# One engine makes the third unit's outputs, one hidden tile goes to the readout's bank, and the fourth unit's preparation stands further on

## What is computed

```
for t in range(S):
    C = f_stab * C + i_stab * outer(v_t, k_t)
    n = f_stab * n + i_stab * k_t
    y_t = sigmoid(o_gate_t) * (C q_t) / max(|n . q_t|, 1)
...
h = x @ w_in
g = where(h >= 1, h, where(h <= -1, 0, (h + 1)**2 / 4))
x = g @ w_out
...
out += P[:, e:e+1] * (max(x @ w1[e], 0) @ w2[e])
```

## Time and profile before

| | us |
|---|---|
| median of 3 runs (lowest, highest) | 923.47 (922.88, 923.96) |
| the profiled execution | 923.94 |
| span of its instructions | 921.8 |
| TensorE busy | 914.6 |
| VectorE busy | 594.1 |
| ScalarE busy | 464.6 |
| GpSimd busy | 617.8 |

### The profile page before, as it was taken

How to read it: one execution, slowest core, us unless ns; L and a number is a source line. 1 busy time by engine, 2 the same in 40 slices (tenths; PEclk the granted TensorE clock), 3 DMA queues, 4 the chain that set the end, 5 groups by cost and what they waited for, 6 DMA issues and landing times.

```text
span 921.8 us, 16392 instructions
## 1 busy us (share of the span) xinstructions
PE 914.6 (99%) x6091; PEld 902.2 (98%) x6091; DVE 594.1 (64%) x1130; ACT 464.6 (50%) x951; POOL 617.8 (67%) x642
## 2 busy tenths in 40 slices
PE   9999999999999999999999999999999999999998
PEld 7899999999999999999999999999999999999998
DVE  7665444447867888866666666666666666666665
ACT  4655545448864445454444445444445444445442
POOL 6963555454786666777777677767776777777652
PEclk9999999999999999999999999999999999999999
DMA  8904324001110111111111111111111111111102
GB/s 263 302 27 115 93 61 104 32 2 38 38 54 22 38 38 38 38 39 59 38 53 38 38 38 38 49 51 44 46 38 38 39 38 60 38 52 38 38 1 86
DMA packets 27599, 53.02 MB, mean 58 GB/s; under 512 B 2304, under 2 KB 15584, under 8 KB 27264
## 3 DMA queue, kind: packets, MB, share of 16 engines
q1 hardware_dynamic: 25984, 46.13, 17.2%
q10 hardware_dynamic: 1440, 5.77, 1.6%
q0 software_dynamic: 96, 0.07, 0.0%
HBM read 49.92 MB, written 2.04 MB: 56 GB/s over the span
## 4 chain that ended last, share of the span: by engine, by line
PE 64%; DVE 1%; issue 0%; ACT 0%; DVEq 0%
PE bank L1680 33%; PE bank L1657 30%; DVE acc L1291 0%; DVE prob L1262 0%; DVE rowsum L1260 0%; DVE prob L1272 0%; DVE h_lo L1308 0%; DVE c L1327 0%; DVE c L1317 0%; DVE acc L1295 0%; ACT h_hi L703 0%; PE bank L1628 0%; ACT h_hi L698 0%; DVE rowinv L1261 0%; DVE colinv L1270 0%
## 5 line engine op out<-in xcount | busy, mean ns | idle before, releaser
L1657 PE MATMUL bank<-xo,wu 128*128 128x384 f32 (+1 forms) x1792 | 377.5, 338 | 0.7 <-DVE s L1311 0.5
L1657 PEld LDWEIGHTS bank<-xo,wu 128*128 128x128 f32 (+1 forms) x1792 | 306.6, 188 | 1.4 <-DVE s L1311 0.7
L1295 DVE SCALAR_TENSOR_TENSOR acc<-bank,prob,acc 128x320 f32<-128x320 f32 x336 | 184.6, 549 | 143.2 <-PE bank L1680 141.7
L1680 PE MATMUL bank<-wd_hi,h_hi 128*128 128x320 f32 x768 | 232.7, 311 | 0.9 <-POOL h_lo L754 0.9
L1680 PE MATMUL bank<-wd_lo,h_hi 128*128 128x320 f32 x768 | 231.3, 309 | 0.0
L754 POOL TENSOR_TENSOR h_lo<-r,h_hi 128x384 fp32r<-128x384 f32 x192 | 194.3, 1031 | 53.2 <-ACT r L704 53.1
L754 POOL TENSOR_TENSOR wu<-raw_up,wu 128x512 fp32r<-128x512 f32 (+1 forms) x128 | 145.6, 1168 | 104.0 <-ACT wu L500 98.7
L703 ACT ACTIVATE h_hi<-c 128x384 fp32r<-128x384 f32 x192 | 100.3, 523 | 185.2 <-DVE c L1317 141.8
L1680 PE MATMUL bank<-wd_hi,h_lo 128*128 128x320 f32 x768 | 174.9, 309 | 0.0
L1680 PEld LDWEIGHTS bank<-wd_hi,h_hi 128*128 128x128 f32 x768 | 144.7, 188 | 1.0 <-issue 0.9
L1680 PEld LDWEIGHTS bank<-wd_lo,h_hi 128*128 128x128 f32 x768 | 145.0, 189 | 0.0
(11 more groups left out here) (154 smaller groups left out, 1307.6 us busy)
## 6 DMA issues: line engine op xcount, KB each, us to landing
raw_up<-ups SPq DMA_DIRECT2D x32, 512.0 KB, 3.5
raw_down<-downs SPq DMA_DIRECT2D x32, 320.0 KB, 2.9
rw<-rows SPq DMA_DIRECT2D x11, 480.0 KB, 6.9
qk_s<-qk SPq DMA_DIRECT2D x12, 416.0 KB
fb<-factors SPq DMA_DIRECT2D x8, 512.0 KB, 6.1
m_raw<-up_down ACTq DMA_DIRECT2D x2, 1440.0 KB, 11.1
result<-acc SPq DMA_DIRECT2D x12, 160.0 KB, 1.9
decb<-factors SPq DMA_DIRECT2D x18, 80.0 KB
```

Of the source, the lines that this page charges most:

```text
L1295: ins = stt(acc[:, unit, :], bank_, prob[:, unit, ex:ex + 1], acc[:, unit, :], ALU.mult, ALU.add)
L1657: last = mm(ring_bank(q, b), a, m, start=(i == 0 and k in (0, 1, 4)), stop=(i == len(parts) - 1), skip_group_check=True)
L1680: last = mm(ps_t[n % RING][:, 0:DM], h[half + f][:, cols], w_[w][:, f, :], start=(i == 0), stop=(i == len(parts) - 1))
```

## The change

Five edits, all in the first 60 us.

**The third unit's outputs.** VectorE makes them alone (`last_outputs`): it multiplies the heads' outputs in PSUM by the gate, makes the denominator's reciprocal, multiplies by it and copies the last 64 columns (semaphore `last_twice`). GpSimd's `over_den(0, 2)` and ScalarE's `twice(2, 2)` go. VectorE's `last_decays(2)` and the fourth unit's first scan no longer stand ahead of it. The first rows are VectorE's queue there in the kernel before, then now. `den` and `rden` are the denominators, bank 7 holds the third unit's readout, `dlast` is what `last_decays` makes.

```diff
--- before
+++ after
@@ -43,3 +43,3 @@
 LOADS = (0, 1, 3, 6, 11, FT1)
-LATE = {0: (4,), 1: (5,), 2: (6, 7), 3: (8,), 4: (9,), 7: (10, 11), 8: (12,), 9: (13,), 12: (14,), 13: (15,)}
+LATE = {1: (4,), 2: (5,), 3: (6,), 4: (7,), 5: (8,), 6: (9,), 7: (10, 11), 8: (12,), 9: (13,), 12: (14,), 13: (15,)}
 FREE = 5
@@ -247,4 +247,4 @@
     ps_decb = bank[7]
-    ps_late = bank[2]
-    ps_late_dE = bank[2][0:QR, P:P + U * H]
+    ps_late = bank[0]
+    ps_late_dE = bank[0][0:QR, P:P + U * H]
     ps_turn_of = (bank[5], bank[3], bank[4])
@@ -258,5 +258,9 @@
 
+    def hidden_bank(g, f):
+
+        return ps_o if (g, f) == (0, 2) else ps_h[f % 2]
+
     def activated(g, f):
 
-        return ps_h[f % 2][:, 0:GN] if g == 0 else gact[:, f % 2, :]
+        return hidden_bank(g, f)[:, 0:GN] if g == 0 else gact[:, f % 2, :]
 
@@ -605,3 +610,2 @@
             turn_hi(xa_turned, 1, ps_turn_of[1], P, xa_hi)
-            twice(2, 2)
             turn_hi(xa_turned, 2, ps_turn_of[2], 2 * P, xa_hi)
@@ -639,3 +643,3 @@
                             act.wait_ge(g1, s - 1)
-                        nc.scalar.activation(vhalf[:, f % 2, :], ps_h[f % 2][:, 0:GN], ACT.Relu,
+                        nc.scalar.activation(vhalf[:, f % 2, :], hidden_bank(g, f)[:, 0:GN], ACT.Relu,
                                              bias=0.5, scale=0.5).then_inc(raised, 1)
@@ -881,3 +885,2 @@
             mlp_piece(0)
-            over_den(0, 2)
             pool.wait_ge(dE_ready, 1)
@@ -909,3 +912,3 @@
                         if r == 3:
-                            if ga == 1 and i == 0:
+                            if ga == 1 and i == 1:
                                 pool.wait_ge(dE_ready, 2)
@@ -917,5 +920,7 @@
             def mlp_piece_at(f):
-                if f < 2:
-                    return
-                for q in ((4, 5, 6, 7) if f == 2 else LATE.get(f, ())):
+                if f == 2:
+                    pieces = range(TABLES // 2, TABLES)
+                else:
+                    pieces = [q for q in LATE.get(f, ()) if q >= TABLES]
+                for q in pieces:
                     mlp_piece(q)
@@ -1100,2 +1105,21 @@
 
+            def last_outputs(o):
+
+                i = GT - 1
+                h = o[:, 0:WO].rearrange("p (h d) -> p h d", h=H)
+                dve.wait_ge(heads_out, GT)
+                nc.vector.tensor_scalar(den[:, i, :], h[:, :, D], -1.0, 1.0, ALU.mult, ALU.max).then_inc(den_step, 1)
+                dve.wait_ge(sigmoid_ready, GT)
+                tt(h[:, :, 0:D], h[:, :, 0:D], rw[:, i, 2, :].rearrange("p (h d) -> p h d", h=H), ALU.mult).then_inc(og_r_ready, 1)
+                dve.wait_ge(den_step, 2 * GT - 1)
+                stt(den[:, i, :], h[:, :, D], 1.0, den[:, i, :], ALU.mult, ALU.max).then_inc(den_step, 1)
+                dve.wait_ge(den_step, 2 * GT)
+                nc.vector.reciprocal(rden[:, i, :], den[:, i, :]).then_inc(rden_ready, 1)
+                dve.wait_ge(rden_ready, GT)
+                dve.wait_ge(og_r_ready, GT)
+                tt(xs[:, i, 0:DM].rearrange("p (h d) -> p h d", h=H), h[:, :, 0:D],
+                   rden[:, i, :].unsqueeze(2).to_broadcast([P, H, D]), ALU.mult).then_inc(xs_ready, 1)
+                dve.wait_ge(xs_ready, GT)
+                nc.vector.tensor_copy(xs[:, i, DM:3 * P], xs[:, i, 2 * P:DM]).then_inc(last_twice, 1)
+
             def spread(u, j):
@@ -1134,13 +1158,10 @@
             outputs(0, 1, ps_o_of[1])
-            last_decays(2)
-            denominators(0, 2, ps_o_of[2])
-            dve.wait_ge(fb_made, 4)
-            dve.wait_ge(vd_ready, 3)
-            decays(1, 0, 0, spread(3, 0))
-            outputs(0, 2, ps_o_of[2])
+            last_outputs(ps_o_of[2])
             turn_lo(xa_hi, 0, ps_turn_of[0], 0, xa_ready)
             turn_lo(xa_hi, 1, ps_turn_of[1], P, xa_ready)
-            add_state(0, 2, ps_o_of[2])
             turn_lo(xa_hi, 2, ps_turn_of[2], 2 * P, xa_ready)
-            decays(1, 0, 1, spread(3, 1))
+            add_state(0, 2, ps_o_of[2])
+            dve.wait_ge(fb_made, 4)
+            dve.wait_ge(vd_ready, 3)
+            decays(1, 0, 0, spread(3, 0))
 
@@ -1188,2 +1209,5 @@
                         add_state(g + 1, i, ps_o)
+                    if first and f == UNIT:
+                        decay_columns(2, ps_late_dE[:, 2 * GH:U * H])
+                        gate_columns(2, ps_late)
                     if lo and 1 <= f <= FT1:
@@ -1193,6 +1217,7 @@
                            ALU.subtract).then_inc(lo1, 1)
-                    if attention and i < GT and r == 2:
-                        if first and f == 2:
-                            decay_columns(2, ps_late_dE[:, 2 * GH:U * H])
-                            gate_columns(2, ps_late)
+                    if first and f == 1:
+                        decays(1, 0, 1, spread(3, 1))
+                    if first and f == 3:
+                        last_decays(2)
+                    if attention and i < GT and (f == 3 if first and i == 0 else r == 2):
                         weigh(g + 1, i, 0)
@@ -1203,3 +1228,3 @@
                         dve.wait_ge(sq1, s + 1)
-                        stt(activated(g, f), ps_h[f % 2][:, 0:GN], 1.0, vhalf[:, f % 2, :], ALU.max, ALU.min).then_inc(g1, 1)
+                        stt(activated(g, f), hidden_bank(g, f)[:, 0:GN], 1.0, vhalf[:, f % 2, :], ALU.max, ALU.min).then_inc(g1, 1)
                     extra(f)
@@ -1460,3 +1485,7 @@
 
-                pe.wait_ge(x_twice, ga * GT + i + 1)
+                u = ga * GT + i
+                if u == GT - 1:
+                    pe.wait_ge(last_twice, 1)
+                else:
+                    pe.wait_ge(x_twice, u + 1 if u < GT - 1 else u)
                 turn_x(i, dst, xa_turned)
@@ -1584,3 +1613,3 @@
                             pe.wait_ge(st_ready, GT)
-                        if first and f >= 2:
+                        if first and f >= 3:
                             pe.wait_ge(lo1, f - 1)
@@ -1588,3 +1617,3 @@
                             pe.wait_ge(g1, s - 1)
-                        first_product(ps_h[f % 2], f, m_hi, m_lo, m_st, g * GN, wait_x_lo).then_inc(h1, 1)
+                        first_product(hidden_bank(g, f), f, m_hi, m_lo, m_st, g * GN, wait_x_lo).then_inc(h1, 1)
                     if f == 0 and not first:
@@ -1598,7 +1627,11 @@
                     if attention and i < GT:
-                        if first and f == 1:
+                        if first and f == 2:
+                            pe.wait_ge(wt_ready, 2 * GT + 2)
+                            weights(g + 1, 0)
+                        if first and f == 4:
+                            pe.wait_ge(at_ready, 2 * GT + 2)
                             late_columns()
-                        if r == 0:
-                            if first and i == 0:
-                                pe.wait_ge(wt_ready, 2 * GT + 2)
+                        if r == 0 and not (first and i == 0):
+                            if first and i == 1:
+                                pe.wait_ge(iT_ready, len(PARTS))
                             weights(g + 1, i)
@@ -1607,3 +1640,3 @@
                             if first and i == 0:
-                                pe.wait_ge(dE_ready, 2)
+                                pe.wait_ge(lo1, 3)
                             heads(g + 1, i, ps_o)
```

7 lines of the change are left out of this document (4 added, 3 removed).

## The result

The changed kernel takes **934.86 us** in the median of three executions (934.11, 934.86, 939.06), the kernel before 923.21 us in the same comparison: a ratio of 1.0127, 95% interval 1.0095 to 1.0159. One further execution, of 4829 us, was disturbed and is left out; with it the median is 936.96. In a second comparison it took 935.63 us in the median (934.04 to 937.66, ratio 1.0118, 1.0093 to 1.0142). The sign was forecast, the size was not: 928.5 us, range 926.8 to 930.6.

A forecast was written before the change was run, and what follows sets the result against it. TensorE, busy 914.6 of 921.8 us, bounds the kernel, so only its waits count. Step 5's lateness of 4.99 us on the profiled 923.94 gives 928.9, less 0.47 to the median: 928.5 us, range 926.8 to 930.6.

The forecast's parts named there:

- The sign: Whole kernel: the change makes it slower, chance 0.90; same 0.07, faster 0.03.
- Step 3's product: First layer: TensorE waits 0.4 us for VectorE's remainder of tile 1 before this product.
- `heads(1, 0)`: Fourth unit's readout: TensorE waits 1.7 us for VectorE's `weigh`, starting at 39.52, 0.38 us later than before.
- step 5's product: TensorE waits 4.2 us on a chain from step 4's product through piece 7; this product starts at 50.32, 4.99 us late.
- the +5.0 us of the sum: Lateness of step 5's product, +4.99 us, added to the profiled execution of 923.94 us.
- the bounds that it names: On the sum: 0.3 less for earlier ScalarE pieces, 0.4 less for overlapping VectorE rows, 0.6 more at step 8.
- A copy of 64 columns until about 25.8 ... every value in this range is hidden: Third unit's outputs: VectorE's copy ends while TensorE's dummies run until 26.42, so the transposes start 0.86 us earlier.
- A slow clock as a rival: After the 4.2 us wait TensorE returns at 1.2 GHz, costing 0.8 to 1.9 us: 929.3 to 930.4; shared chance 0.26.
- all behind step 9 is only shifted: From step 9 on all queues are as before and only shifted, adding no further time.
- The rival *a blocked `last_decays`: GpSimd's `m_lo` holds VectorE's `last_decays`, making `weigh` 0.9 to 1.4 us later: 929.4 to 929.9; shared chance 0.26.

The follow-up runs named there:

- early-`weigh` kernel with the columns from PSUM: Changed kernel with GpSimd's piece 7 in step 4, `weigh(1, 0)` back in step 2, last 64 columns made from PSUM: 922.29 us, ratio 0.9991.
- the last one of the fourth set: Changed kernel with columns from PSUM, fourth unit's gate in step 3, `last_decays` behind `weigh`, GpSimd's piece 7 in step 4: 922.83 us, ratio 0.9996.
- its two variants of the third set: Changed kernel with columns from PSUM, plus either 6 and 16 dummy matmuls in the two later waits (935.40 us) or the fourth unit's gate in step 3 (934.72 us).
- The fastest kernel: Changed kernel with piece 7 in step 4, `weigh(1, 0)` in step 2, columns from PSUM, fourth unit's gate in step 3: 922.01 us, ratio 0.9979.
- the first set: Here: changed kernel with 6 dummy matmuls ahead of `heads(1, 0)` and 16 behind the late columns: 932.67 us, ratio 1.0091.
- the third: Here: changed kernel with columns from PSUM, 6 dummy matmuls ahead of the readout and 16 ahead of step 5's product: 935.40 us, ratio 1.0120.

## Why the prediction was right and wrong

- **The sign and the queues: right.** Step 3's product waited 0.31 and 0.46 us (forecast 0.4), `heads(1, 0)` 1.66 and 1.62 (1.7), step 5's product 4.16 in both profiles (4.2), released by `at` and `ht_lo` as said. Against an undisturbed start these make the +5.0 us of the sum. The experiments that remove them one by one confirm the last two as causes. Two small slips in the working change nothing: TensorE reaches the readout at 37.7 by its own terms (34.88 + 2.8), not 37.8, and the bounds that it names give 927.8 to 929.1, not 927.5 to 929.5.
- **"A copy of 64 columns until about 25.8 ... every value in this range is hidden": wrong, the first failing step.** The edit was priced at a gain of 0.86 us by the size of the copy and by its nearest row, `xs`. That row reads PSUM; the copy reads and writes SBUF, while GpSimd has two pieces in a row to make. It took 3.32 us, and the transposes waited 2.85 us for it. VectorE's chain moves as a whole with the start, so the later waits keep their size and this loss is carried on in full. I had weighed contention for `last_decays` alone and read in the earlier trace rows only how GpSimd's `m_lo` (2.33 us) is stretched. VectorE's scan of two SBUF operands had been issued 0.4 us before that `m_lo` (22.49 and 22.89 in the changed kernel's rows, where `m_lo` also takes 2.32). The `dlast` row, 0.97 us at 23.55, is the other case: it was issued behind that `m_lo` and ends (24.52) 0.07 us after it (24.45). The Trainium skill, "SBUF — State Buffer", section "Who interferes with whom", says that a copy in VectorE's two-port mode shares its ports with GpSimd and that the one issued first blocks the other for a whole instruction. The trace agrees that the two hold each other up; no row shows which mode the copy ran in. On order and length it shows something else: the copy was issued 0.09 us ahead of `m_lo` by the rows (26.76, 26.85) and was yet the one held, through three GpSimd products and not one. GpSimd's DMA instruction ran from 26.28 to 26.83 there, and in the kernel with the first edit alone (copy at 26.50, DMA instruction until 26.60) it is the same; whether that gave GpSimd the ports was not tried.
- **A slow clock as a rival and not as a part of the sum: wrong, the second failing step.** It had a price of 0.8 to 1.9 us for the long wait, and the measured one, 1.4 in the second comparison's profile, lies in that (in part by luck: other kernels of the study lost 1.8 to 2.5 us behind the same wait). But it came twice, also after the wait that I had not seen, and I gave it a share of 0.26 together with another rival and added it nowhere.
- **The sum, mended.** For the profiled execution the forecast was a span of 921.8 + 4.99 = 926.8 us. Its three dummies ahead of the transposes start at 26.33 and not at 25.54, since the first nine dummies of that execution took 4.21 us for the 3.71 of the earlier trace rows and what follows kept the distance: 0.79, a difference of executions (another kernel of the study starts them at 25.73). The transposes are 2.93 later than 0.79 + 26.42: the copy. From the first product to step 5's it is 24.01 us (31.36, 55.37), forecast 22.68 (27.64, 50.32): 1.43 of slow clock and 0.1 less than forecast, so the queues themselves are right within 0.1. Behind step 5 the second slow stretch gives 1.43. That is 926.8 + 0.79 + 2.93 + 1.43 - 0.10 + 1.43 = 933.3; measured are 932.4. The last 0.9 is a wait that goes: TensorE's waits behind 70 us in the kernel before list

```profile
PE bank L1680 <- POOL h_lo L754: 0.9, 1, 0.9
PE bank L1657 <- DVE s L1311: 0.5, 1, 0.5
```

  and in the changed kernel the second is there (0.5, for `s`) and the first is not. I had said that all behind step 9 is only shifted; it is not, by this 0.9. The early-`weigh` kernel with the columns from PSUM lacks this wait too (922.29), though it is ahead of the kernel before and not behind it; the last one of the fourth set has it (922.83).
- **The rival *a blocked `last_decays`*: there, but small in the change.** `dlast` took 0.71 us in both profiles, because GpSimd's products were nearly done when it came. In the change with the columns from PSUM and its two variants of the third set it took 0.68, 1.53 and 2.23 us. Its price, 0.9 to 1.4 us in the prediction, was 2.2 us of wait and some 6 us of time where it was at its worst.
- **What I didn't see: the terms don't add.** The kernel with the copy mended took 935.5, with the gate's DMA then mended 934.7, and only with `dlast` moved 928.4. Each cover that is removed shows the next late thing: a wait for a DMA that doesn't move with the queues, then a row on shared ports, and both times a slow stretch at the fourth unit's readout, where the change has none in the second comparison's profile.
- **The range** was too narrow for the same two reasons: its upper end of 930.6 held one slow stretch, and nothing for the copy.

What stays open: why single executions of the changed kernel reach 937 to 939 us with a mean clock of 0.987 to 0.989. The profile of one shows the fall at about 20 us, which puts the first product 2.85 us later (34.21, 31.36), and a slow stretch behind the readout that adds 1.9 us up to step 5's product (25.90 us from the first product, against 24.01): together nearly all of the 4.9 us between the two profiles. The others have no profile. Nor did a run tell why `h_lo` is late in one kernel and not in another, or why a slow stretch is long in one execution and short in another.

## What to carry to other kernels

For each VectorE instruction that an edit adds or moves, ask where its operands are and which GpSimd instructions stand in the same microseconds: with all operands in SBUF, price it from its own length up to several of GpSimd's products (0.19 to 2.23 us for `dlast`, 0.31 to 3.34 for the copy), and if the same numbers are still in PSUM, read them there (0.36 us against 3.32) or give the copy to ScalarE (0.26). Price a wait of TensorE of some microseconds as the wait plus a slow stretch: behind waits of 2.8 to 4.7 us it cost 1.4 to 4.0 us here, and behind the wait of 1.6 us before the readout nothing in two profiles and some 3 us in one. And before an edit puts an instruction behind an engine's own later product, follow the four queues round: a chain that comes back to the engine where it started sets a distance that no faster engine shortens.

## What the runs showed that was not expected

- **The kernel before has two levels of its own.** Of its 78 executions in the comparisons 16 took 927.2 to 928.9 us with a mean clock of 0.993 or 0.994, the others nearly all 922.7 to 924.3 with 1.000: 4.9 us for a clock fall that the edits don't cause. The fastest kernel has it too. Its windows in an execution of 928.14 us:

```profile
10.00:20.00 10.00, 10.00 (x116) 8.80 (x114) 8.71 (x15) 4.59 (x8) 9.12 (x16) 0.97 0.95 285
20.00:30.00 10.00, 10.00 (x57) 9.14 (x57) 4.10 (x13) 3.98 (x11) 8.42 (x10) 0.50 1.00 396
30.00:40.00 10.00, 9.80 (x54) 8.80 (x54) 6.39 (x13) 5.66 (x13) 4.66 (x7) 0.85 0.82 261
```

  TensorE was busy 10.00 of 10.00 us before the clock fell, with small matmuls (42 columns in the readouts, where the dummies have 512), and 0.50 is its lower level. In the profile of the kernel before it is just as busy there, 10.00 of 10.00 us with 119 matmuls, and the clock stays at 1.00, so these rows don't tell the two cases apart. A median of few runs of this kernel may be off by up to 4.9 us, and single times are only compared at a like clock.
- **Dummies help only in part.** With 16 in the last wait the clock stayed up behind it (1.00 from 42 to 60 us in the first set), but six in the readout's wait did not keep it up in the third.
- **A held row can pass over the gaps between GpSimd's instructions.** The copy stood through three products and the held `dlast` (2.23 us) through parts of three; neither got in where one product ended and the next began (28.22 and 28.63; 37.25 and 37.66). But both got in at the end of an `m_lo` though an `m_st` followed it (29.99, 39.02), and in the early-`weigh` kernel with the columns from PSUM `dlast` got in at the first such end (issued at 38.14, ended at 39.22; `m_lo` until 39.14). What is alike in every profile of the study, for the copy and for each `dlast` of 16x64 that took 0.3 us or more, is the end: 0.06 to 0.09 us after some product of GpSimd has ended. Which of them lets VectorE in is not shown.
